# Attention with both heads of a pair in one step: scores in row groups, one row maximum, v beside zeros

## The reference

```python
def _attn_ref(q, k, v):                       # q, k, v: (4, 8, 576, 64)
    scores = scale * np.matmul(q, k.transpose(0, 1, 3, 2))
    mask = block_i >= block_j                 # blocks of 64 tokens
    scores = np.where(mask, scores, -1000000000.0)
    scores = scores - np.max(scores, axis=-1, keepdims=True)
    attn = np.exp(scores)
    attn = attn / (np.sum(attn, axis=-1, keepdims=True) + 1e-09)
    return np.matmul(attn, v)

def _moe_ref(x, w_gate, w_val, w_out):        # x: 2304 tokens x 512
    return (1.0 / (1.0 + np.exp(-(x @ w_gate))) * (x @ w_val)) @ w_out

def _moe2_ref(x, domain_probs, w1, w2):       # 4 experts, all computed
    return sum(p[:, e:e + 1] * (np.maximum(x @ w1[e], 0.0) @ w2[e]) for e in range(4))
```

## Time and profile before

| | us |
|---|---|
| median of 3 runs (lowest, highest) | 1462.43 (1461.35, 1463.72) |
| the profiled execution | 1460.69 |
| its span in the profile | 1458.9 |
| first scores | 15.09 |
| first matmul of the later layers | 276.06 |

### The profile page before, as it was taken

One profiled execution on the slowest core, in us unless ns is written; L12 is line 12 of the kernel. 1 busy time (PEld: TensorE's weight loads), 2 busy tenths in 40 slices (PEclk: granted clock), 3 DMA queues, 4 the chain that ended last, 5 costly groups with the idle time before them and its releaser, 6 DMA issues.

```text
span 1458.9 us, 22264 instructions
## 1 busy us (share of the span) xinstructions
PE 1412.2 (97%) x7816; PEld 1285.4 (88%) x7816; DVE 899.9 (62%) x1551; ACT 727.1 (50%) x1472; POOL 432.2 (30%) x675
## 2 busy tenths in 40 slices
PE   5998998999999999999999999999999999999999
PEld 4877777899998989899999989899899999899897
DVE  4887889677545546376774636364757646364453
ACT  4777888656444324254663535253546436243341
POOL 3555667544201212021541112021234312022100
PEclk8999999999999999999999999999999999999999
DMA  7787887122214122132232222131232312131302
GB/s 167 187 205 179 212 217 183 50 81 77 83 32 143 58 73 73 44 97 77 73 89 86 87 73 73 44 102 44 73 97 63 101 58 73 44 102 44 101 8 80
DMA packets 201198, 136.76 MB, mean 94 GB/s; under 512 B 66144, under 2 KB 170624, under 8 KB 201088
## 3 DMA queue, kind: packets, MB, share of 16 engines
q1 hardware_dynamic: 199504, 134.42, 33.2%
q10 hardware_dynamic: 1520, 0.89, 0.3%
q0 software_dynamic: 64, 0.04, 0.0%
HBM read 97.55 MB, written 9.44 MB: 73 GB/s over the span
## 4 chain that ended last, share of the span: by engine, by line
PE 84%; DVE 8%; SPq 3%; DMA 2%; issue 1%; ACT 1%; POOL 1%; DVEq 0%; ACTq 0%; POOLq 0%
PE pb L929 26%; PE pb L931 25%; PE pb L930 25%; DVE ptl L335 2%; PE pt L400 2%; SPq L146 2%; DVE nmax L313 2%; PE ov L425 1%; PE st L388 1%; PE st L436 1%; SPq L138 1%; PE st L389 1%; DVE x1p L348 1%; DMA craw<-in_moe_w_dram 1%; DVE qtl L341 1%
## 5 line engine op out<-in xcount | busy, mean ns | idle before, releaser
L929 PE MATMUL pb<-xch,ul 128*128 128x384 f32 x1176 | 398.7, 339 | 5.2 <-DVE cb L863 3.7
L931 PE MATMUL pb<-xch,uh 128*128 128x384 f32 x1176 | 393.6, 335 | 0.0
L930 PE MATMUL pb<-xcl,uh 128*128 128x384 f32 x1176 | 393.3, 334 | 0.0
L720 POOL TENSOR_TENSOR us<-ura 128x256 f32<-128x256 f32 x84 | 62.3, 742 | 850.7 <-DVE ul L664 832.6
L929 PEld LDWEIGHTS pb<-xch,ul 128*128 128x128 f32 x1176 | 220.7, 188 | 23.1 <-issue 16.1
L931 PE MATMUL pb<-ch,rh 128*128 128x512 f32 x576 | 224.6, 390 | 0.0
L930 PE MATMUL pb<-cl,rh 128*128 128x512 f32 x576 | 224.5, 390 | 0.0
L929 PE MATMUL pb<-ch,rl 128*128 128x512 f32 x576 | 224.1, 389 | 0.0
L930 PEld LDWEIGHTS pb<-xcl,uh 128*128 128x128 f32 x1176 | 220.9, 188 | 0.4
L931 PEld LDWEIGHTS pb<-xch,uh 128*128 128x128 f32 x1176 | 220.7, 188 | 0.0
L832 DVE TENSOR_TENSOR cl<-craw,ch 128x512 fp32r<-128x512 f32 x132 | 91.5, 707 | 113.8 <-ACT ch L767 113.6
(11 more groups left out here) (104 smaller groups left out, 2553.6 us busy)
## 6 DMA issues: line engine op xcount, KB each, us to landing
ura<-in_moe_w_dram SPq DMA_DIRECT2D x96, 256.0 KB, 3.1
craw<-in_moe_w_dram SPq DMA_DIRECT2D x96, 256.0 KB, 2.8
ura<-in_moe_w_gate_dram SPq DMA_DIRECT2D x36, 256.0 KB, 3.3
ura<-in_moe_w_val_dram SPq DMA_DIRECT2D x36, 256.0 KB, 3.3
craw<-in_moe_w_out_dram SPq DMA_DIRECT2D x36, 256.0 KB, 3.2
qhl<-qth SPq DMA_DIRECT2D x32, 144.0 KB, 3.2
qhl<-qtl SPq DMA_DIRECT2D x32, 144.0 KB, 3.1
qlh<-qtl SPq DMA_DIRECT2D x32, 144.0 KB, 3.1
```

The costliest lines, as they stand in the source:

```text
L720: nc.gpsimd.tensor_tensor(us[:, 0, :], a21, a22, ALU.add).then_inc(us_ok, 1)
L929: nc.tensor.matmul(acc, lhs[1], rhs[0], start=start, stop=False, skip_group_check=True)
L930: nc.tensor.matmul(acc, lhs[0], rhs[1], start=False, stop=False, skip_group_check=True)
L931: return nc.tensor.matmul(acc, lhs[0], rhs[0], start=False, stop=stop, skip_group_check=True)
```

## The change

A step now handles tile j of *both* heads of a pair: 80 steps in place of 160.

- **Scores.** The stacking and its DMAs are gone. `qth`, `qtl`, `kth`, `ktl` have two buffers each and are read in place: head 0 in partitions 0 to 63, head 1 in 64 to 127. Three products (low x high, high x low, high x high) for each head, K=64, alternating between the two row groups, and a mask for each head (none for tile 0). A tile takes two banks of `st`, one for each head: 0 and 1 for tiles 0 and 2, 2 and 3 for tiles 1 and 3, all four for tile 4.
- **Row maximum.** One reduction gives both heads' maxima; the exponentials stay one for each head.
- **Transposes.** Nine units a pair instead of twelve; those of tiles 0 and 1, and two blocks of tile 4 of each head, take both heads into one bank. They run three steps (of a pair) behind the scores.
- **Output.** `vh` and `vl` hold (v of head 0, zeros, v of head 1). Columns 0 to 127 put head 0's output in the lower half of `ov` and zeros in the upper, columns 64 to 191 the reverse; three products of both heads are summed there, and one ScalarE copy evicts the pair.
- **Preparation** of the next pair's q and k stands in steps 1 and 2 of each pair, in `ov`. The later layers' `with_...` functions are called twice a step.

```diff
+PAIRS = HEADS // 2
+STEPS = 5 * PAIRS
+TAIL = 6
...
-    LAG_T, LAG_HI, LAG_LO, LAG_PV, LAG_OHI, LAG_OLO = 6, 5, 6, 13, 15, 16
-    PV_PARTS = {0: (0,), 1: (1,), 2: (2, 3, 4)}
-    INVERSE = {0: 3, 3: 5}
+    LAG = 3
+    UNITS_OF = {0: [(BOTH, 0, 1)], 1: [(BOTH, 0, 2)], 2: [(ONE, 0, 3), (TWO, 0, 3)], 3: [(ONE, 0, 4), (TWO, 0, 4)],
+                4: [(ONE, 0, 3), (BOTH, 3, 5), (TWO, 0, 3)]}
+    EARLY = (1, 2, 3)
+    INVERSE = {1: 2, 2: 1, 3: 1, 4: 1}
+    SCORES_AT = (0, 2, 0, 2)
...
         def prep_of(t):
-            p = t // 5 + 3
-            return p if exists(t) and t % 5 == 4 and p < HEADS else None
+            m, what = t // 5 + 1, t % 5 - 1
+            return 2 * m + what if exists(t) and what in (0, 1) and m < PAIRS else None
...
             for t in range(STEPS + TAIL):
-                if t == 4:
-                    prep(2)
-                if prep_of(t - 1) is not None:
-                    prep(prep_of(t - 1))
-                if exists(t):
+                of = units(t - LAG)
+                if exists(t) and t % 5 in EARLY:
                     exp(t)
-                if exists(t - LAG_HI):
-                    transposed_hi(t - LAG_HI)
-                with_act(act, t, qk_ps)
-                if (t - LAG_OHI) % 5 == 0 and exists(t - LAG_OHI):
-                    output((t - LAG_OHI) // 5)
+                for unit in of[:2]:
+                    transposed_hi(t - LAG, *unit)
+                if prep_of(t) is not None:
+                    prep(prep_of(t))
+                if t % 5 == 0 and t >= 10:
+                    output(t // 5 - 2)
+                with_act(act, 2 * t, qk_ps)
+                if exists(t) and t % 5 not in EARLY:
+                    exp(t)
+                for unit in of[2:]:
+                    transposed_hi(t - LAG, *unit)
+                with_act(act, 2 * t + 1, qk_ps)
...
-                nc.vector.tensor_reduce(nmax[:, t % BODY:t % BODY + 1], scores_view(j), AX.X if j < 4 else AX.XY,
-                                        ALU.max, negate=True).then_inc(nmax_ok, 1)
+                if j < 4:
+                    of, axes = st[:, SCORES_AT[j]:SCORES_AT[j] + 2, 0:width(j)], AX.X
+                else:
+                    of, axes = st[:, :, 0:HALF].rearrange("p (a h) n -> p h a n", h=2), AX.XY
+                nc.vector.tensor_reduce(nmax[:, t % BODY, :], of, axes, ALU.max, negate=True).then_inc(nmax_ok, 1)
...
-                    nc.tensor.matmul(out, qhl[u][:, h, P * j:P * j + P], keys, start=True, stop=False)
-                    nc.tensor.matmul(out, qlh[u][:, h, P * j:P * j + P], keys, start=False, stop=(hi < P * j + 64))
+                after(pe, exp_ok, 2 * t if j == 0 else 2 * t - 2)
+                for i in range(1 if j < 4 else 2):
+                    if i == 1:
+                        pe.wait_ge(exp_ok, 2 * t)
...
+                    for x, (left, right) in enumerate(((qtl, kth), (qth, ktl), (qth, kth))):
+                        for h in range(2):
+                            rows = slice(64 * h, 64 * h + 64)
+                            mm = nc.tensor.matmul(out[h], left[u][rows, queries], right[u][rows, keys], start=(x == 0),
+                                                  stop=(x == 2 and not masked), skip_group_check=True)
...
+            def output(n, chunks):
+                u = n % 2
+                if chunks[0] == 0:
+                    pe.wait_ge(pt_lo, PER_PAIR * n + PER_PAIR)
+                    pe.wait_ge(v_lo, 2 * n + 2)
+                    after(pe, o_ok, n)
+
+                    pe.wait_ge(prep_lo, 2 * min(n + 3, PAIRS))
...
+                        for x, (left, half) in enumerate(((vl, 0), (vh, 1), (vh, 0))):
+                            for h in range(2):
...
+                                mm = nc.tensor.matmul(out, left[u][:, c, h:h + 2, :].rearrange("p h d -> p (h d)"),
+                                                      moving, start=(c == 0 and x == 0 and h == 0),
...
+                if exists(t) and j in EARLY:
+                    scores(t)
+                if j == 0 and n >= 2:
+                    output(n - 2, (3, 4))
+                for unit in of[:2]:
+                    transpose_probs(t - LAG, *unit)
+                if prep_of(t) is not None:
+                    prep(prep_of(t))
+                if j == 4 and n >= 1:
+                    output(n - 1, (1,))
+                with_pe(pe, 2 * t, exp_ok, pt_lo)
+                if exists(t) and j not in EARLY:
+                    scores(t)
+                if j == 3 and n >= 1:
+                    output(n - 1, (0,))
+                if j == 4 and n >= 1:
+                    output(n - 1, (2,))
+                for unit in of[2:]:
+                    transpose_probs(t - LAG, *unit)
```

More of the change, by code:

```diff
@@ L189, in _ @@
             load(sp, 0, q_v, qn, q_in)
-            sp.wait_ge(prep_lo, 1)
-            stack_q(0, 0)
             next_q(0)
-            stack_q(0, 1)
+            next_k(0)
             load(sp, 0, v_v, vn, v_in)
-            next_k(0)
-            pair(1, early=True)
-            for n in range(2, PAIRS):
-                pair(n, last=(n == PAIRS - 1))
-                with_sp(sp, n)
+            for m in range(1, PAIRS):
+                if m + 1 < PAIRS:
+                    next_q(m)
+                sp.wait_ge(v_lo, 2 * m)
+                load(sp, m, v_v, vn, v_in)
+                if m + 1 < PAIRS:
+                    next_k(m)
+                if m >= 3:
+                    pair_out(m - 3)
+                with_sp(sp, m)
@@ new lines, in _ @@
+            for t in range(STEPS + TAIL):
+                n, j = divmod(t - 1, 5)
+                if exists(t - 1) and j in INVERSE:
+                    pool.wait_ge(rinv_ok, len(INVERSE) * n + sorted(INVERSE).index(j) + 1)
+                    pool.sem_inc(pool_on, 1)
+                    for of in range(t - INVERSE[j], t):
+                        normalize(of)
+                if exists(t) and t % 5 == 1:
+                    for i in range(2):
+                        split_v(t // 5, i)
+                for i in range(2):
+                    with_pool(pool, 2 * t + i)
@@ new lines, in prep, with transposed_hi @@
+            def prep(p):
+                act.wait_ge(prep_ps, p + 1)
+                after(act, qk_ps, 5 * (p // 2 - 1))
+                nc.scalar.activation(prep_tile(p, 0), prep_place(p)[:, 0:S], ACT.Copy,
+                                     scale=SCALE if p % 2 == 0 else 1.0).then_inc(prep_hi, 1)
+            def transposed_hi(t, unit, heads, c0, c1):
+                n, j = divmod(t, 5)
+                act.wait_ge(pt_ps, unit + 1)
+                after(act, o_ps, n - 1 if j < 3 else n)
+                nc.scalar.activation(transposed(0, t, heads, c0, c1), unit_ps(unit, heads, c0, c1), ACT.Copy)\
+                    .then_inc(pt_hi, 1)
@@ L352, in _ @@
             for t in range(STEPS + TAIL):
-                ends = exists(t - 1) and (t - 1) % 5 + 1 in INVERSE.values()
-                if exists(t):
+                of = units(t - LAG)
+                ends = exists(t - 1) and (t - 1) % 5 in INVERSE
+                if exists(t) and t % 5 in EARLY:
                     row_max(t)
+                for unit in of[:1]:
+                    transposed_lo(t - LAG, *unit)
                 if ends:
                     plus_eps(t - 1)
-                if exists(t - LAG_LO):
-                    transposed_lo(t - LAG_LO)
+                for unit in of[1:2]:
+                    transposed_lo(t - LAG, *unit)
@@ L390, in scores @@
-                w = hi - lo
-                nc.tensor.matmul(st[:, bank, w - 64:w], maskrow[:, :], ones[:, :], start=False, stop=True)\
-                    .then_inc(qk_ps, 1)
-            def transpose_probs(t):
-                j, g = t % 5, t // 5
-                pe.wait_ge(norm_ok, t + 1)
-                for unit, chunks in units(j):
-                    after(pe, pt_lo, 6 * g + unit - 1)
-                    for i, c in enumerate(chunks):
-                        mm = nc.tensor.transpose(pt[:, unit % 2, P * i:P * i + P], probs[g % 2][j][:, P * c:P * c + P],
-                                                 ident[:, :])
-                    mm.then_inc(pt_ps, 1)
@@ new lines, in scores, with transpose_probs @@
+                mm.then_inc(qk_ps, 1)
+            def transpose_probs(t, unit, heads, c0, c1):
+                pe.wait_ge(norm_ok, 2 * t + heads.stop)
+                after(pe, pt_lo, unit - 1)
+                i = 0
+                for h in range(heads.start, heads.stop):
+                    for c in range(c0, c1):
+                        mm = nc.tensor.transpose(pt[:, unit % 2, P * i:P * i + P],
+                                                 probs[h][t % 5][:, P * c:P * c + P], ident[:, :])
+                        i += 1
+                mm.then_inc(pt_ps, 1)
@@ L434, in prep @@
                 pe.wait_ge(got, 48 * (p // 2) + 48)
+                if p > 1:
+                    pe.wait_ge(prep_lo, p)
```

(2 more changed lines are left out.)

337 lines of the change are left out of this document (134 added, 203 removed).

## The result

The changed kernel takes 1520.01 us in the median (1518.22 to 1522.28), beside 1461.89 for the kernel before on the same chip: 1.0407 times as long, 95% interval 1.0394 to 1.042. The forecast was 1524 us, range 1478 to 1560, and slower with 0.91. The profiled execution took 1519.78 us against 1460.69.

A forecast was written before the change was run, and what follows sets the result against it. TensorE was taken to bound the kernel before, a closed queue loop the changed one: pairs of 20.3 us end the attention 59.5 us later, 2.6 more behind it, sum 1523, with 1.7 for the median 1524; range 1478 to 1560.

The forecast's parts named there:

- The walk through the queues: Engine queues over one pair: last low part at 11.2 us, then 8.0 us of TensorE, a loop of 19.2 us.
- The clock: TensorE, underused early in each pair, drops to the 1.2 GHz level: 0 to 2.2 us a pair, 1.1 taken.
- The start: Kernel start: first scores at 9.4 us instead of 15.09 without the stacking transfer, gaining 5.7 us once.
- The sum: Whole kernel: attention ends 59.5 us later, work behind it adds 2.6, together +62 us, giving 1523.
- the signs that it named: Changed profile: period near 20 us, waits for tile 2's maximum and low subtracts, clock under 1.00, first scores near 9.4.
- The scores: Score matmuls on TensorE: 3.8 us a pair, loads one after another, columns of two row groups side by side.
- The lower bound of 1.9: Score matmuls on TensorE: 1.9 us a pair if both loads and columns of the two row groups overlap.
- The test named for tile 3: Tile 3's six score matmuls: about 0.64 us if loads bound them, 1.1 if nothing overlaps, 0.55 if both do.
- TensorE is the bound: Attention of the kernel before: TensorE busy 14.75 of 15.22 us a pair, VectorE close behind.
- TensorE's sum of 16.8 us: TensorE's work per pair after the change: 14.75 + 2.2 + 0.6 - 0.8, forbidding a gain unless row groups overlap fully.
- the loop: Each pair's output waits for its last low part, the next pair's transposes for that output: 19.2 us.
- TensorE's sum alone: Rival for the attention: queues run far enough ahead, period 16.8 us, +21 us, 1483; chance 0.13.

The follow-up runs named there:

- after: The changed kernel itself, both heads of a pair handled in one step: 1520.01 us, 1.0407 times the kernel before.
- e1: The changed kernel with 24 identity transposes a pair added in TensorE's two holes of step 2, into a bank nobody reads: 1507.05 us, 1.0308.
- e8: The changed kernel with all 128 rows in every score matmul, summing both heads, so the result is off: 1527.96 us, 1.045.
- e11: e9 with the sum and reciprocal of tiles 0 and 1 moved from behind the maximum of tile 3 into step 1: 1483.72 us, 1.0148.
- e6: The kernel before with the low product of the output issued twice, 16 matmuls a pair more: 1468.58 us, 1.0046.
- e7: e5 plus tile 2's scores and maximum in step 1, tile 4's scores before output row 1, first output block awaiting only its own units: 1484.97 us, 1.0165.
- e2: The changed kernel with the halves of q and k shrunk to 16 of 576 columns from the third pair on: 1508.18 us, 1.0309.
- e4: The changed kernel with tile 2's maximum behind tile 1's on VectorE, its exponential ahead of q's high half on ScalarE: 1507.07 us, 1.03.
- e3: The changed kernel without the output's product of v low with the probabilities' high part, 16 matmuls a pair less: 1502.38 us, 1.0275.
- e5: The changed kernel with the output's rows 3 and 4 and its eviction moved from step 0 to step 1: 1522.78 us, 1.0417.
- e9: e7 with tile 3's scores between step 2's first two transposes and its maximum behind step 2's first low part: 1497.28 us, 1.0253.
- e12: e11 with a filler of 3 and 9 identity transposes in its TensorE holes: 1479.05 us, 1.0137.

## Why the prediction was right, and where it was not

**The walk through the queues held link by link.** From 84.03 us as t = 0:

| | walked | measured |
|---|---|---|
| exponential 0 starts | 2.5 | 2.5 |
| high copies of 512 done | 4.9 | 4.9 |
| low half of q done | 6.4 | 6.4 |
| maximum of tile 2 done | 7.2 | 7.2 |
| exponentials of tile 2 done | 8.2 | 8.2 |
| high half of k done | 9.7 | 9.7 |
| last high copy done | 10.3 | 10.5 |
| last low part done, output starts | 11.2 | 11.2, 11.3 |
| TensorE's stretch | 8.0 + 1.1 for the clock | 8.8 |
| period | 20.3 | 20.1 |

The prices from the nearest forms carried this: 0.156 + 1.04 ns a column gives 0.82 us for a maximum of 640, and 1.35 for 1152. After shows (beside the earlier trace rows, by line and shape, 0 to 330 us):

```profile
L318 DVE TENSOR_REDUCE nmax<-st 128x2 f32<-128x1152 f32 x16 | 21.7, 1355 | 10.2 <-PE st L393 10.1
...
L318 DVE TENSOR_REDUCE nmax<-st 128x2 f32<-128x640 f32 x16 | 13.0, 815 | 0.0
```

**The clock** was the right mechanism and nearly the right size: e1 gives 1.2 us a pair, 1.1 was taken. **The start** came at 9.40, as said. **The sum** was 62 us, 59.1 were measured: the first matmul of the later layers was put at 335 us and came at 333, and the work behind it at 2.6 and came to 2.1. Its terms held one by one, so little of this is luck: the first scores of the second pair came 15.1 us behind those of the first (15 said), those of the third another 20.0 behind (19 said), and the rest took 288.5 us (292 said, with 8 of it for the later layers). Of the signs that it named one did not show as named: the view prints no wait of TensorE ahead of the first output.

**The scores were mis-sized.** 3.8 us a pair was taken, loads as the floor. The rates that e8 sets side by side give both in parallel. From the first score matmul of each tile to its mask, after took 0.76 + 0.55 + 0.86 + 0.90 = 3.1 us in this pair, of which 0.15 is the lower clock in tile 3. The lower bound of 1.9 had counted loads alone: two matmuls of 448 columns take 0.20 us, two of 320 take 0.15, for their columns, and the first two of a tile behind other work 0.10 more. The test named for tile 3 (0.64, 1.1 or 0.55) was badly chosen, since its six matmuls, 0.71 us at the full clock in e11, lie near two of the three; the 64 columns of tile 0 tell them apart.

**"TensorE is the bound" was the step that failed,** and with it TensorE's sum of 16.8 us and the sentence that this alone forbids a gain. e6 refutes the first. The sum also took 2.2 us for the added output matmuls, where the walk's own terms for them (1.9, 1.5, 1.35 and 1.35, 6.1 us in all) stand only 1.7 above the 4.4 of the kernel before; e1 has 6.3 at the full clock. For the whole, e11's pair of 17.32 us holds 1.67 us of waits that the view prints (0.34 for the first, then 1.08 and 0.25), so TensorE's work is 15.65 us at most. It cost the forecast little, because the loop and not the sum set the period; the rival "TensorE's sum alone", 1483, lay near where e7 came out, but there too waits and not the sum made up the rest.

**The worth of a link was overrated, in the experiments though not in the forecast.** The walk named one way round the loop, and other ways are not much shorter, as the waits that came up show: through the bank of the transposes (e2), through the low half of q (e4), through exponential 4 (e3, e5), through the reciprocal and GpSimd (e9). Their lengths were not measured one by one. That is why one edit gave 12 to 18 us, and four together (e7) 35.

What stays open: e12 has pairs of 17.3 us with no wait over 0.26 us in TensorE's view and 1.3 us of filler. What holds them above the 15.2 of before is not shown, nor whether another order brings the rest back. The start gained by the missing stacking is in all of these kernels, and none of them that handles both heads in a step came below the kernel before.

## What to carry to other kernels

When an edit merges steps or shortens the distance between a producer and its consumer, walk every in-order queue through one period with durations from the trace: which instruction stands behind which decides more than the sum of any engine. Before taking a link out of such a loop, list the other ways round it and their lengths; the gain ends at the second longest. And don't call TensorE the bound from its busy share: compare distances between starts with the known rate, or give it harmless extra work and see whether the time moves.

## What the runs showed of the hardware

**Idle TensorE is paid twice.** A hole of 2.1 us, ahead of it one of 1.2, was followed by some 3 us at the 1.2 GHz level in the midst of full work; 24 transposes a pair that compute nothing, in idle time, made the kernel 13 us faster (e1). With 12 a pair (e12) the granted clock rose from 0.97 to 1.00, and eleven pairs of the profile took 4.9 us less.

**Going from all rows to row groups costs 0.1 to 0.2 us.** In after the scores of tile 4 follow outputs in which all 128 rows work; in e8 both use all rows, and the change comes at the mask instead. TensorE's timeline of after, then of e8:

```profile
99.95 0.40 PE L434 MATMUL ov<-pzh,vh 128*128 128x256 f32 x2
100.28 0.41 PE L387 MATMUL st<-kth,qtl 64*128 64x288 f32 x2
```

```profile
103.96 0.40 PE L434 MATMUL ov<-pzh,vh 128*128 128x256 f32 x2
104.20 0.42 PE L387 MATMUL st<-kth,qtl 128*128 128x288 f32 x2
...
105.52 0.43 PE L387 MATMUL st<-kth,qth 128*128 128x288 f32 x2
105.88 0.20 PE L393 MATMUL st<-ones,maskrow 64*128 64x64 bf16 x2
```

Two outputs of 256 columns take 0.24 us from start to start; with the change behind them 0.33. Two scores of 288 take 0.26 (104.20 to 104.46 in e8), with the change 0.36. Behind transposes it costs more: from the five of q to the scores of tile 2 after takes 0.63 us (86.81 to 87.44) and e8 0.47 (111.99 to 112.46). Scores stand in four places of a pair, three of them behind transposes, which makes an estimated 0.6 us of TensorE's time. The way back was not separated; two masks and the change back take 0.13 us (101.18 to 101.31), where one mask takes 0.04 to 0.06 in the kernel before, so it is small. The prediction, which counted ten changes a pair, had cited the Trainium skill (TensorEngine Tiling (Array Packing), Key Properties), that a change of tiling mode drains TensorE, without a row for it; these rows agree and give it a price.
